# Batch 0's prologue: no filler matmuls, half the turned copies on VectorE, later weight loads

## The reference

```python
X = np.fft.rfft(x, axis=1)
F = (filt_r + 1j * filt_i)[None, :, :]
x = np.fft.irfft(X * F, n=x.shape[1], axis=1)      # (4, 3008, 256)
x = x.reshape(B * S, D)
g = np.maximum(x @ w_in, 0.0) ** 2                 # d_ff 2048
x = g @ w_out
g, val = x @ w_gate, x @ w_val                     # d_ff 1536
out = (g / (1 + np.exp(-g)) * val) @ w_out2
```

## Time and profile before

| | us |
|---|---|
| median of 3 runs (lowest, highest) | 2320.13 (2318.55, 2321.81) |
| the profiled execution | 2318.55 |
| its span | 2316.7 |
| PE busy, share | 2301.8, 99% |
| DVE busy, share | 1537.5, 66% |
| ACT busy, share | 1208.7, 52% |
| POOL busy, share | 63.3, 3% |

### The profile page before, as it was taken

The page is one execution under the profiler, slowest core; times in us unless marked ns, Lnnn a source line. Parts: engine busy times, 40 slices in busy tenths (PEclk is TensorE's granted clock), DMA queues, the critical chain, the costliest instruction groups (busy, mean ns, idle before and its releaser), DMA issues.

```text
span 2316.7 us, 30842 instructions
## 1 busy us (share of the span) xinstructions
PE 2301.8 (99%) x10719; PEld 1908.3 (82%) x10719; DVE 1537.5 (66%) x2515; ACT 1208.7 (52%) x2271; POOL 63.3 (3%) x126
## 2 busy tenths in 40 slices
PE   9999999999999999999999999999999999999999
PEld 6788888888888888888888878888888888888887
DVE  5657755566555665555545877777777777777776
ACT  5656655565555554444444445555555555555554
POOL 1100000000000000000000000000000000000000
PEclk9999999999999999999999999999999999999999
DMA  9524333333333323001002101001011011010000
GB/s 320 154 89 127 105 109 92 90 105 104 99 90 95 110 87 118 25 24 38 24 19 73 39 13 37 17 21 37 1 37 37 1 37 37 1 37 28 10 19 19
DMA packets 88346, 146.15 MB, mean 63 GB/s; under 512 B 10092, under 2 KB 39500, under 8 KB 88192
## 3 DMA queue, kind: packets, MB, share of 16 engines
q1 hardware_dynamic: 79760, 129.88, 17.3%
q0 software_dynamic: 8432, 14.31, 2.3%
HBM read 97.49 MB, written 46.66 MB: 62 GB/s over the span
## 4 chain that ended last, share of the span: by engine, by line
PE 96%; ACT 1%; DVE 1%; DMA 1%; issue 1%; SPq 0%; ACTq 0%; DVEq 0%
PE psum L1394 31%; PE psum L1396 31%; PE psum L1395 31%; PE psum L1509 2%; ACT turned L790 1%; PE psum L1415 1%; DVE m L1087 0%; DMA w<-w_full 0%; DMA b_in<-B_here_scratch 0%; ACT z_raw L790 0%; DMA zq_raw<-z_scratch 0%; DVE m L1092 0%; ACT b_out L790 0%; PE psum L1464 0%; DMA B_here_scratch<-b_out 0%
## 5 line engine op out<-in xcount | busy, mean ns | idle before, releaser
L1170 DVE SCALAR_TENSOR_TENSOR prod<-psum,act_out 128x512 f32<-128x512 f32 (+1 forms) x384 | 261.1, 680 | 464.4 <-ACT act_out L884 464.0
L884 ACT ACTIVATE act_out<-psum 128x512 f32<-128x512 f32 (+1 forms) x384 | 226.3, 589 | 515.8 <-PE psum L1396 515.3
L1394 PE MATMUL psum<-g_hi,m_hi 128*128 128x512 f32 (+1 forms) x768 | 307.2, 400 | 1.8 <-ACT z_raw L790 1.6
L1394 PE MATMUL psum<-v_hi,m_hi 128*128 128x512 f32 (+1 forms) x768 | 297.5, 387 | 0.6 <-DVE v_lo L1073 0.6
L1396 PE MATMUL psum<-g_hi,m_lo 128*128 128x512 f32 (+1 forms) x768 | 297.1, 387 | 0.0
L1396 PE MATMUL psum<-v_hi,m_lo 128*128 128x512 f32 (+1 forms) x768 | 296.2, 386 | 0.0
L1395 PE MATMUL psum<-v_lo,m_hi 128*128 128x512 f32 (+1 forms) x768 | 296.0, 385 | 0.0
L1395 PE MATMUL psum<-g_lo,m_hi 128*128 128x512 f32 (+1 forms) x768 | 295.4, 385 | 0.0
L1073 DVE TENSOR_TENSOR g_lo<-prod,g_hi 128x512 fp32r<-128x512 f32 (+1 forms) x408 | 270.6, 663 | 1.1 <-ACT g_hi L790 1.0
L790 ACT ACTIVATE g_hi<-prod 128x512 fp32r<-128x512 f32 (+1 forms) x408 | 248.5, 609 | 0.8 <-DVE prod L1204 0.8
L1394 PE MATMUL psum<-g_hi,m_out 128*128 128x512 f32 (+1 forms) x576 | 221.8, 385 | 0.4 <-DVE g_lo L1073 0.4
(11 more groups left out here) (125 smaller groups left out, 4027.1 us busy)
## 6 DMA issues: line engine op xcount, KB each, us to landing
filt_in<-filt SPq DMA_DIRECT2D x36, 512.0 KB, 4.0
z_scratch<-z_raw SPq DMA_DIRECT2D x23, 512.0 KB, 2.9
zq_raw<-z_scratch SPq DMA_DIRECT2D x44, 256.0 KB, 3.5
x_in<-x SPq DMA_DIRECT2D x48, 192.0 KB, 2.9
A_scratch<-a_out SPq DMA_DIRECT2D x48, 192.0 KB, 2.1
a_in<-A_scratch SPq DMA_DIRECT2D x36, 256.0 KB, 3.0
B_scratch<-b_out SPq DMA_DIRECT2D x36, 256.0 KB, 2.0
b_in<-B_scratch SPq DMA_DIRECT2D x96, 96.0 KB, 2.6
```

What stands on the lines that cost most here:

```text
L884: nc.scalar.activation(act_out[n % 2][:, 0:w], psum[:, n % 3, 0:w], ACT.Relu).then_inc(relu_done, 1)
L1170: nc.vector.scalar_tensor_tensor(out=prod[n % 2][:, 0:w], in0=psum[:, n % 3, 0:w], scalar=0.0, in1=act_out[n % 2][:, 0:w], op0=ALU.max, op ...
L1394: nc.tensor.matmul(dst, wh, vh, start=start, stop=False, skip_group_check=True)
```

## The change

Three edits, all in the prologue:

1. `warm_up`, its nine calls (16 matmuls), the tile of zeros and its memset go.
2. `copy_t0(u)` for odd u goes from ScalarE to VectorE, ahead of `multiply0(u - 2)`. The semaphore t0_copied becomes one for each engine, and PE's waits look at the one of the unit's parity.
3. The six weight loads of k = 1, 2, 3 are issued after the wait for b0_loaded, ahead of SP's main loop.

```diff
-                if u in (1, 3, 5):
-                    load_w_in((u + 1) // 2)
-                    load_w_out((u + 1) // 2)
             for u in (UPS - 2, UPS - 1):
                 load_b0(u)
             sp.wait_ge(b0_loaded, 16 * UPS)
+            for k in range(1, 4):
+                load_w_in(k)
+                load_w_out(k)
...
             copy_t0(0)
-            copy_t0(1)
             for u in range(UPS):
                 turn0(u)
-                if u + 2 < UPS:
+                if u % 2 == 0 and u + 2 < UPS:
                     copy_t0(u + 2)
...
-            nc.vector.memset(as_f32(zeros[:, :]), 0.0).then_inc(zeros_ready, 1)
...
+            def copy_t0(u):
+                dve.wait_ge(t0_done, u + 1)
+                wait(dve, s2_0_done, u - 2)
+                nc.vector.tensor_copy(flat(a_in[u % 3][:, :, :]), psum[:, 6 + u % 2, :]).then_inc(t0_copied[1], 1)
...
+            copy_t0(1)
             for u in range(UPS):
+                if u % 2 and u + 2 < UPS:
+                    copy_t0(u + 2)
                 multiply0(u)
                 add0(u)
...
-                wait(pe, t0_copied, u - 1)
+                wait(pe, t0_copied[u % 2], u // 2)
...
-                pe.wait_ge(t0_copied, u + 1)
+                pe.wait_ge(t0_copied[u % 2], u // 2 + 1)
...
-            warm_up(8)
             for j in range(PGS):
                 s1_0(j)
-                if j % 2:
-                    warm_up(1)
```

More of the change, by code:

```diff
@@ L220, in build @@
         assert at <= z_raw_at
-        zeros, _ = place(z_raw_at, "zeros", [P, T], F32R)
         b0_in, at = place(W_IN * PIECE * 2, "b0_in", [ROWS, PAIR * G0, D])
@@ L294, in build @@
         warm_ready = sem("warm_ready")
-        zeros_ready = sem("zeros_ready")
         x0_w1_loaded = [sem(f"x0_w1_loaded{k}") for k in range(len(CUTS) - 1)]
@@ L303, in build @@
         t0_done = sem("t0_done")
-        t0_copied = sem("t0_copied")
+        t0_copied = [sem(f"t0_copied{k}") for k in range(2)]
         s2_0_done = sem("s2_0_done")
@@ L802, in copy_t0 @@
                 wait(act, s2_0_done, u - 2)
-                copy(flat(a_in[u % 3][:, :, :]), psum[:, 6 + u % 2, :]).then_inc(t0_copied, 1)
+                copy(flat(a_in[u % 3][:, :, :]), psum[:, 6 + u % 2, :]).then_inc(t0_copied[0], 1)
             def turn0(u):
@@ L1396, in product @@
                 return nc.tensor.matmul(dst, wl, vh, start=False, stop=stop, skip_group_check=True)
[L1399 to L1404, removed]
             def s1_0(j):
```

## The result

The changed kernel took 2337.78 us (median of 4 runs, 2336.01 to 2338.56) against 2319.36 (2318.55 to 2321.81): ratio 1.0077, interval 1.0059 to 1.0094. That is +18.4 us, where +4.0 was forecast. The two profiled spans are 2335.2 and 2316.7 us, 18.5 apart, so the traces can be laid side by side.

The account below looks back on a forecast made before the run. PE bounds the main stages, full from about 74 us, so prologue shifts move the end. Terms -0.5 + 0.2 + 0 + 2.6 + 1.7 = +4.0 us on 2320.13 gave 2324.1 us; 8-in-10 range 2319.7 to 2328.5.

Parts of the forecast that it names:

- Fillers: Step 1: without fillers its first two pieces run at 1.2 GHz, then the clock rises; -0.5 us.
- Rival C: Step 1 stays at 1.2 GHz throughout, ending at 32.3 us instead of 21.3: +11.0 us, 2335.6 in all; chance 9%.
- Copy to VectorE: Loop over units: copies covered by slack except at the loop's end, where the last one delays VectorE; +0.2 us.
- rival D: Loop over units: VectorE becomes the bound, six units cost 5 us, 2329 us in all; chance 4%.
- Out of the loop: Loop's end: weight loads had landed before the last store, and keep_busy holds PE anyway; 0 us.
- Ahead of x_in: Before batch 1's first piece: x_in lands behind six weight loads, ScalarE waits, PE starts later; +2.6 us.
- Clock after the wait: Behind PE's idle time before batch 1's first piece: granted clock falls to half for a stretch; +1.7 us.
- rival A: Batch 1's start: x_in lands before 72 us, so wait and clock terms vanish; -0.3 us, 2319.8; chance 15%.

Follow-up runs that it names:

- e1: Kernel before without its 16 filler matmuls, nothing else changed: 2331.0 us, ratio 1.003.
- e8: Kernel before without fillers, each step 1 matmul taking 192 columns instead of 96 (outputs not the reference's): 2326.01 us.
- e3: Kernel before with only the odd t0 copies moved to VectorE: 2322.15 us, ratio 1.0003; its profiled execution took 2335.15.
- e2: Kernel before with the eight fillers ahead of step 1 kept and those between its pieces removed: 2325.18 us, ratio 1.0012.
- p16: Kernel before with 16 fillers ahead of step 1 instead of eight: 2321.98 us, ratio 0.9996.
- e4: Kernel before with only the six weight loads moved ahead of x_in: 2327.28 us, ratio 1.0015.
- e6: Kernel before with the six weight loads out of the loop, issued after the first four x_in loads: 2317.98 us, ratio 0.9985.
- e9: Kernel before with weight loads ahead of x_in, plus nine unread matmuls on TensorE before batch 1's first piece: 2323.79 us, ratio 1.0004.
- b12: Kernel before with 12 fillers ahead of step 1 instead of eight and weight loads after the first four x_in: 2318.59 us, ratio 0.9956.
- b16: Kernel before with 16 fillers ahead of step 1 instead of eight and weight loads after the first four x_in: 2319.7 us, ratio 0.9986.
- e11: Kernel before without fillers and with weight loads ahead of x_in, all t0 copies on ScalarE: 2336.96 us, ratio 1.0037.
- e10: Kernel before without fillers and with weight loads after the first four x_in: 2330.89 us, ratio 1.0025.

## Why the prediction was wrong, point by point

- **Fillers, forecast -0.5, bounds -0.6 and +0.7: measured +12.8** (10.96 + 1.68, and 0.14 at the loop's start), the step that failed. I took the clock to rise after two pieces "because PE has no gap while it is that slow". It never rose within step 1: e1 does it alone, and next to e8 it shows that an engine without a gap in the profile can stay at the low level with one kind of matmul and leave it with another. Rival C had this place and its price (27.4 us for step 1, measured 27.6), with a chance of 9%; the argument used against it, that PE never idles at that level, was the wrong one. PE did not idle, and the level stayed low all the same. It also left out the transposes behind it, at the low level too. The Trainium skill's warning (TensorE: Matmul & The Clock Gate, section HAM oscillation) pointed to the right outcome, though by load waits, of which e1 and the changed kernel had none within step 1.
- **Copy to VectorE, +0.2: right.** Of the stage's 0.38 the low clock has 0.14, which leaves 0.24; the end of the loop grew by 0.23 in e3. Rounds stayed at 2.61 us, and rival D did not occur.
- **Out of the loop, 0, bounds 0 and -0.5: measured -1.83 in the stage, and -0.37 ahead of it.** Two parts. keep_busy ran at the high level. I had read the 7.30 us of keep_busy as a fixed floor; it was one execution's clock, and in 10 of the 14 traces it takes 5.97. And the round trip got shorter: 57.56 to 64.39 was 6.8 us, and it is 75.21 - 70.17 = 5.0 here, although the weights had landed before the last store in before. With step 1 at the high level it is 6.7 to 7.7 us with the loads in the loop (before, e2, e8, p16) and 5.1 to 5.6 without them (e4, e6, e9, b12, b16). But with step 1 at the low level it was 5.0 us in e1, which has the loads in the loop, and 6.2 in e3. So in the changed kernel the gain can't be put down to this edit. That e6 is no slower than before in spite of the later loads fits the shorter trip.
- **Ahead of x_in, +2.6, bounds 0 and +3.6: measured +5.37 (step 4 to s1(0)).** The mechanism was right, the size was not: x_in was there 13.4 us after SP went on, not 10.8 (14.9 in e4, 13.3 in e9, 12.0 in e11). The first weight load landed 5.2 us after its issue; the next four came 1.3 to 1.4 us apart (512 KB at 369 GB/s take 1.4), and the last 2.2. I divided by 369 GB/s from the loop; DMA moved 336 GB/s from 75.2 to 88.6 us for all queues together. POOL's six tables for batch 1 were landing until 78.2 us, which fits the late first one but was not tested. Of the small terms, the 0.8 us before the first byte and the 1.0 behind the last, no row gives either by itself; with x_in's 0.5 they make 2.3, where such a load alone takes 2.9. From there on the working held: x_hi starts 13.4 us after SP went on instead of 7.9, +5.5, and VectorE gives 0.15 of it back.
- **Clock after the wait, +1.7, bounds 0 and +2.5: measured +2.31.** Right: 0.50 until 95.2 us, and with PE kept busy in e9 the clock is 1.00 there.
- **The range** (2319.7 to 2328.5) rested on the forecast and rival A and left C out. It would have held edit 3 alone (2327.3) and not edit 1.

What stays open: what decides in a given run whether eight fillers bring the clock up. They start at 1.46 us in before and in e3 alike; in before the level rises at 4.75 us, during the last of them, in e3 not before the loop, and nothing that the two traces show ahead of 4.75 tells them apart. Why the round trip is shorter in most traces with the weights out of the loop, and why e1 has it short without that, was not separated either.

## What to carry to other kernels

A phase of small matmuls can keep TensorE busy to 100% in the profile and still not leave 1.2 GHz (27.6 us here); read the distance of starts, not the busy share or the first rows of the granted clock, and don't take away filler matmuls from such a phase without measuring. A transfer that the next stage waits for goes ahead of prefetches in the queue, not behind them: the same six loads cost 6 us ahead of x_in (e11 over e10) and no wait behind it. Where one profile shows two things ending together, check in a second execution which of them is fixed, and look at more than three or four runs of a kernel before trusting its median.

## What was not expected of the hardware

- Step 1 with 96 columns an instruction (0.213 us each) ran 27.6 us without a gap at the low level; with 192 columns the level rose at 9.76 us of the span (e8).
- After eight fillers the level rose between 4.7 and 6.5 us of the span in five traces, in e2 and e6 within step 1, and not before the loop in a sixth (e3).
- The same program with fillers ends above 2332 us in 23 of 97 runs, median 2322.9; e3's trace, the only one of such a run, has step 1 at the low level.
- Idle gaps of 0.82 and 0.74 us in a phase of small matmuls were followed by the low clock (e2), while 1.34 us ahead of s1(0), behind 512-column products, were not the earlier trace rows. The wait between 1334 and 1355 us, 1.6 to 2.3 us long, was followed by it in five of fourteen traces.
